# Pooling an image for attention: the second column addition moves from VectorE into TensorE's pooling matmuls

## What is computed

```python
# q (1, 12288, 128), kv (1, 384, 32, 128), w_sr (128, 128); r = 4, C = 128
kv_pool = kv.reshape(B, H // r, r, W // r, r, C).mean(axis=(2, 4))   # mean over 4x4 pixels: 96 x 8 = 768 keys
kv_flat = kv_pool.reshape(B, -1, C) @ w_sr
k = v = kv_flat
s = scale * (q @ k.transpose(0, 2, 1))
a = softmax(s)
x = a @ v
# then, with d_ff = 2048 in both:
h = x @ moe_w_in;   y = (h * clip(h + 3, 0, 6) / 6) @ moe_w_out
h = y @ moe2_w_in;  out = where(h >= 1, h, where(h <= -1, 0, (h + 1)**2 / 4)) @ moe2_w_out
```

## Time and profile before

| what | value |
|---|---|
| runs | 1310.63, 1313.53, 1312.01 us; median 1312.01 |
| profiled execution | 1311.85 us in all, span 1310.1 us |
| instructions | 17871 |
| TensorE matmul busy | 1282.6 us, 98% of the span |
| VectorE busy | 1221.4 us, 93% |
| ScalarE busy | 1141.8 us, 87% |
| GpSimd busy | 431.0 us, 33% |
| HBM | 16.84 MB read, 6.29 MB written |

### The profile page before, as it was taken

The page is one execution under the profiler, slowest core; times in us unless marked ns, Lnnn a source line. Parts: engine busy times, 40 slices in busy tenths (PEclk is TensorE's granted clock), DMA queues, the critical chain, the costliest instruction groups (busy, mean ns, idle before and its releaser), DMA issues.

```text
span 1310.1 us, 17871 instructions
## 1 busy us (share of the span) xinstructions
PE 1282.6 (98%) x5826; PEld 1071.5 (82%) x5826; DVE 1221.4 (93%) x1168; ACT 1141.8 (87%) x1314; POOL 431.0 (33%) x201
## 2 busy tenths in 40 slices
PE   7897999999999999999999999999999999999998
PEld 6785888888888888888888888888888888888876
DVE  5797999999999999999999999999999999999898
ACT  3776989989989899899899998998989989988997
POOL 1654325135143152350441522504415225132000
PEclk9998999999999999999999999999999999999999
DMA  9111220311202202202112022021120220210000
GB/s 337 19 33 32 58 57 9 65 47 19 64 18 46 56 8 64 52 12 64 24 40 56 8 64 56 8 64 30 34 57 9 62 55 2 57 37 21 9 9 17
DMA packets 118500, 58.23 MB, mean 44 GB/s; under 512 B 103104, under 2 KB 104256, under 8 KB 118208
## 3 DMA queue, kind: packets, MB, share of 16 engines
q1 hardware_dynamic: 117408, 57.64, 19.0%
q10 hardware_dynamic: 1056, 0.13, 0.1%
HBM read 16.84 MB, written 6.29 MB: 18 GB/s over the span
## 4 chain that ended last, share of the span: by engine, by line
PE 90%; DVE 6%; ACT 1%; POOL 1%; issue 1%; SPq 1%; DMA 1%; ACTq 0%
PE ps L898 37%; PE ps L874 37%; PE ps L779 7%; PE ps L766 7%; DVE g_lo L664 2%; DVE gate L658 2%; SPq L283 1%; PE ps L811 1%; PE ps L819 1%; POOL probs L343 1%; DVE negmax L570 1%; PE ps L827 0%; DMA kv_sb<-in_kv 0%; ACT gate L474 0%; DVE gate L653 0%
## 5 line engine op out<-in xcount | busy, mean ns | idle before, releaser
L664 DVE TENSOR_TENSOR g_lo<-gate,g_hi 128x1024 fp32r<-128x1024 f32 x384 | 549.5, 1431 | 7.7 <-ACT g_hi L488 7.7
L658 DVE SCALAR_TENSOR_TENSOR gate<-gate,ps 128x1024 f32<-128x1024 f32 x384 | 463.5, 1207 | 12.5 <-ACT gate L482 10.6
L488 ACT ACTIVATE g_hi<-gate 128x1024 fp32r<-128x1024 f32 x384 | 402.7, 1049 | 1.4 <-DVE gate L658 1.2
L348 POOL TENSOR_TENSOR pt_lo<-pt,pt_hi 128x1024 fp32r<-128x1024 f32 x66 | 158.8, 2407 | 623.1 <-ACT pt_hi L430 623.1
L898 PE MATMUL ps<-g_hi,w_hi 128*128 128x512 f32 x768 | 301.4, 392 | 2.7 <-DVE g_lo L664 1.3
L898 PE MATMUL ps<-g_hi,w_lo 128*128 128x512 f32 x768 | 299.5, 390 | 0.0
L898 PE MATMUL ps<-g_lo,w_hi 128*128 128x512 f32 x768 | 299.4, 390 | 0.0
L343 POOL TENSOR_TENSOR probs<-probs,rinv 128x768 f32<-128x768 f32 x96 | 223.9, 2342 | 70.4 <-DVE rinv L579 70.4
L474 ACT ACTIVATE gate<-ps 128x1024 f32<-128x1024 f32 x192 | 196.9, 1025 | 55.2 <-PE ps L874 55.1
L472 ACT ACTIVATE gate<-ps 128x1024 f32<-128x1024 f32 x192 | 196.1, 1021 | 50.5 <-PE ps L874 49.3
L482 ACT ACTIVATE gate<-gate 128x1024 f32<-128x1024 f32 x187 | 198.6, 1062 | 5.9
(11 more groups left out here) (75 smaller groups left out, 1403.2 us busy)
## 6 DMA issues: line engine op xcount, KB each, us to landing
pt<-turned_p SPq DMA_DIRECT2D x352, 96.0 KB, 2.2
out<-out_sb SPq DMA_DIRECT2D x94, 64.0 KB, 1.8
kv_sb<-in_kv SPq DMA_DIRECT2D x11, 512.0 KB, 7.9
q_in<-in_q SPq DMA_DIRECT2D x88, 64.0 KB, 2.2
w_raw<-in_moe_w_in SPq DMA_DIRECT2D x2, 1024.0 KB, 14.3
kv_sb<-in_kv SPq DMA_DIRECT2D x2, 256.0 KB, 11.9
out_sb<-in_q SPq DMA_DIRECT2D x1, 256.0 KB, 12.4
q_in<-in_q SPq DMA_DIRECT2D x1, 256.0 KB, 11.7
```

Source lines behind the costliest of these rows:

```text
L348: nc.gpsimd.tensor_tensor(piece(pt_lo, g), piece(pt, g), piece(pt_hi, g).bitcast(F32), ALU.subtract).then_inc(pt_lo_done, 1)
L488: nc.scalar.activation(g_hi[:, n % RING, :], gate[:, n % RING, :], ACT.Copy).then_inc(g_hi_done, 1)
L658: nc.vector.scalar_tensor_tensor(out=gate[:, n % RING, :], in0=gate[:, n % RING, :], scalar=6.0 if mlp == 1 else 1.0, in1=hidden, op0=ALU. ...
L664: nc.vector.tensor_tensor(g_lo[:, n % RING, :], gate[:, n % RING, :], g_hi[:, n % RING, :].bitcast(F32), ALU.subtract).then_inc(g_lo_done, 1)
```

## The change

`col_sum` and `sum_cols` go. `pool_rows` waits for `halves_summed` instead and issues, for each group, two matmuls that read the two remaining columns straight from `kv_sb` and accumulate in one place of PSUM. `keep_warm(6)` behind the parts of the first two thirds becomes `keep_warm(2)`. `values_low(0)` moves from behind `sum_halves(7)` to behind `keys_low(0)`, ahead of `sum_halves(7)`. The semaphore `cols_used` is renamed `pooled`. `keys_low(1)` and `values_low(1)` stay behind all sums.

```diff
         with ExitStack() as first:
             kv_sb = sb("kv_sb", [P, KVROWS * KVW], F32, first)
-            col_sum = sb("col_sum", [P, KVROWS, WG, C], F32, first)
...
             for j in range(KVROWS):
                 keys = slice(j * KJ, (j + 1) * KJ)
-                act.wait_ge(cols_used, j + 1)
+                act.wait_ge(pooled, j + 1)
...
-            def sum_cols(m):
-                j, g, count = parts[m]
-                part = image(m).rearrange("p (g b c) -> p g b c", b=POOL, c=C)
-                dve.wait_ge(halves_summed, m + 1)
-                nc.vector.tensor_tensor(col_sum[:, j, g:g + count, :], part[:, :, 0], part[:, :, 1],
-                                        ALU.add).then_inc(cols_summed, 1)
-
...
             for m in range(PARTS):
                 sum_halves(m)
-                if 0 < m < PARTS - 2:
-                    sum_cols(m - 1)
                 if m == 6:
                     keys_low(0)
-                if m == 7:
                     values_low(0)
-                if m == PARTS - 3:
-                    sum_cols(m)
-            sum_cols(PARTS - 2)
-            sum_cols(PARTS - 1)
             keys_low(1)
             values_low(1)
             first_q_low(0)
...
             def pool_rows(m):
                 j, first, count = parts[m]
-                pe.wait_ge(cols_summed, m + 1)
+                pe.wait_ge(halves_summed, m + 1)
                 for g in range(first, first + count):
-                    last = nc.tensor.matmul(pooled_keys(j)[:, g * rows:(g + 1) * rows], col_sum[:, j, g, :], pool_m[:],
-                                            start=True, stop=True)
+                    for e in range(2):
+                        at = j * KVW + (g * POOL + e) * C
+                        last = nc.tensor.matmul(pooled_keys(j)[:, g * rows:(g + 1) * rows], kv_sb[:, at:at + C], pool_m[:],
+                                                start=(e == 0), stop=(e == 1))
                 if first + count == WG:
-                    last.then_inc(cols_used, 1)
+                    last.then_inc(pooled, 1)
...
             for m, (j, first, count) in enumerate(parts):
                 pool_rows(m)
-                if m == PARTS - 1:
+                if j < KVROWS - 1:
+                    keep_warm(2)
+                elif m == PARTS - 1:
                     turn_first_q(0)
-                elif j < KVROWS - 1:
-                    keep_warm(6)
```

More of the change, by code:

```diff
@@ L189, in build_program @@
         const_step, const_done = sem("const_step"), sem("const_done")
-        halves_summed, cols_summed, cols_used, pooled_copied = (
-            sem("halves_summed"), sem("cols_summed"), sem("cols_used"), sem("pooled_copied"))
+        halves_summed, pooled, pooled_copied = sem("halves_summed"), sem("pooled"), sem("pooled_copied")
         kt_done, kt_hi_done, kt_lo_done = sem("kt_done"), sem("kt_hi_done"), sem("kt_lo_done")
```

## The result

The changed kernel takes 1322.37 us (median of 4 runs, 1321.56 to 1323.68) against 1311.32 us for the kernel before (4 runs, 1310.18 to 1313.53): the ratio is 1.0083, with a 95% interval of 1.0066 to 1.0101. It is 11 us slower. The forecast was 1312.9 with 1322.0 as the upper end; the time lies inside what rival 1 gave, 1321.4 to 1323.6. The profiled execution of the changed kernel is the longest of its four (1323.68 us), so the shifts read from its trace come out slightly larger than that of the medians.

The account below looks back on a forecast made before the run. TensorE, busy 98% of the span, was taken as the bound. -1.57 + 0.07 + 0.27 + 1.71 gave +0.48 us, or +1.2 with a fixed clock rise; the middle, +0.9 on 1312.01, gave 1312.9 us, range 1310.6 to 1322.0.

Parts of the forecast that it names:

- rival 1: TensorE's clock stays low through all pooling: four transposes end 9.4 us late, 1321.4 to 1323.6 us; chance 0.42, full form 0.25.
- if the clock rises with `keys_and_values(0)` as it does now: Condition of the sum: TensorE's clock rises near the first keys and values and holds, giving +0.48 us; chance 0.48.
- the slow L766 above: First scores: up to 2.2 us more if L766's first twelve passes are slow too; left out of the range.
- A fall in the last third: Last third, 3.4 us of only 32-column passes: the clock falls back there, the same loss in another place.
- Step 1: Start of TensorE: it waits only for the first sum of halves, so starts at 5.90, 1.57 us earlier.
- Step 2: First third: 40 passes for 40 take the same 8.45 us; two transposes cover less of the keys' copy, 0.07 lost.
- Step 3: Second third: 40 passes for 40 at the fast pace; two transposes cover 0.21 of the 0.48 us copy, 0.27 lost.
- Step 4: Last third: 16 more pool passes with nothing taken away cost 1.71 us; accumulation charged zero.
- Step 5: VectorE: losing 5.2 us of additions gains nothing beyond the earlier start; the moved `values_low(0)` costs zero.
- The sum of the first five steps: Prologue total: +0.48 us, or +1.2 if the clock rises at 15.93 in any case; middle +0.9.
- Rival 2: Pooling: doubled pool passes raise the clock sooner than transposes do, gaining at best 2.8 us (1309.2); chance 0.10.
- Rival 3: Last third: a quarter of the 16 passes' 1.71 us were waits for `cols_summed`; about zero or -0.3 us, within the 0.48 case.

Follow-up runs that it names:

- before_warm2: Kernel before with two transposes in place of six behind each part of the first two thirds, nothing else: 1314.78 us, ratio 1.002.
- before_fill128: Kernel before with each part's six filling transposes replaced by three real float32 matmuls of the identity with itself, six 128-column passes: 1312.53 us, ratio 1.0003.
- before_fill32: Kernel before with each part's six filling transposes replaced by three float32 matmuls with the pooling matrix, six 32-column passes: 1320.43 us, ratio 1.007.
- after_early34_w4: Changed kernel with 34 transposes ahead of the first part and four in place of two behind each part: 1313.11 us, ratio 1.0002.
- before_dup_warm2: Kernel before, column sums kept, each pool matmul issued twice without accumulating, two transposes in place of six: 1324.63 us, ratio 1.0092.
- before_values: Kernel before with only the values' low part of the first third moved ahead of the sum of part 7: 1312.16 us, ratio 0.9999.
- before_early34: Kernel before with 34 transposes ahead of the first part: 1311.21 us, ratio 0.9992.
- after_early18: Changed kernel with 18 more transposes ahead of the first part, in TensorE's wait for the first load: 1322.44 us, ratio 1.0081.
- after_warm6: Changed kernel with six transposes in place of two behind each part of the first two thirds: 1321.88 us, ratio 1.0074, runs in two groups.

## Why the prediction was wrong

- **The step that failed** is the condition of the sum, "if the clock rises with `keys_and_values(0)` as it does now", together with the 0.52 against 0.42 that I gave it. It rested on a coincidence in the earlier trace rows: L838's first pass began at 15.71 us in TensorE's timeline and the pace changed at about 15.92, so I gave its columns part of the credit. In the changed kernel keys and values ran in full at 14.62 and at 24.77 and the clock did not rise. What the runs showed in its place: the rise hangs on the filling passes. Taking four of six away is enough to lose it (before_warm2). With as many passes in the same 2.13 us a part it comes at 18.4 us when the filling ones move 128 columns and only near 34.3 when they move 32 (before_fill128, before_fill32). In the changed kernel it comes at 39 in place of 15.9; with the clock high through the pooling, 9 of the 11 us go (after_early34_w4). L838 in the timeline of the kernel before:

```profile
15.71 0.71 PE L838 MATMUL ps<-pooled_t,w_sr_sb 128*128 128x256 f32 x2
```

- **What the trace had said against it.** "TensorE was without a gap from 7.47, yet stayed slow until 15.9, so issuing alone does not raise it" was the right reading. A change that thins out wide passes should then have been taken to keep the clock low until a run showed otherwise.
- **Rival 1** priced the result well. It put the end of the four transposes at 33.6 (34.41), with 1.8 us for keys and values (2.05), 6.5 for the last third (6.67), 0.9 for the transposes (0.91) and up to 2.2 more for the scores; 0.6 was measured there (3.01 against 2.40), and 0.7 ahead of them (34.41 to 36.97 against 24.20 to 26.09), where the last third's keys, values and keep-warm transposes ran slow; the prediction had no term for these. The total of 1321.4 to 1323.6 holds the 1322.37.
- **The range** left out the upper half of that rival ("the slow L766 above") and so missed the time by 0.4 us. A case that had 0.25 of chance in its full form should have stood in it with its own upper bound. A fall in the last third, which the prediction named as the same loss in another place, was seen as well, in after_early34_w4 at about 24.7.
- **Step 1** (earlier start) was right: 6.09 against 5.90, the first load being 0.18 later in this execution. **Step 2** held: 8.53 us from the first pass to keys, against 8.45 + 0.07, with 0.08 of waiting at 14.53.
- **Step 3** held in form: 40 passes for 40, but at 0.203. Its 0.27 us for a copy that two fast transposes do not cover could not show: at the slow pace two transposes take 0.48, as long as the copy needs. No run has two transposes a part at the high pace through this third.
- **Step 4** held: 16 more passes, no charge for accumulation. before_dup_warm2 has the same pace without it, and after_early34_w4 gives 3.49 us at the high pace for the 3.42 of the forecast.
- **Step 5** held at the low pace: from 6.09 to 39.98 the chain of the changed kernel never touches VectorE. The moved values cost nothing by themselves in before_values. Behind its last sum VectorE now waits 5.88 us for keys. With the clock up the step would not hold without limit: in before_early34 TensorE waits 1.10 us for a column sum.
- **The sum of the first five steps** (+0.48 to +1.2) was never measured by itself. The nearest is after_early34_w4 beside before_early34, 1.67 us later at the first scores with 16 added transposes among them.
- **Rival 2** fell: with twice the pool passes the rise came later, not sooner. The rule named with it, in the Trainium skill, "TensorE: Matmul & The Clock Gate", Part 4 (PE-mode transpose), is that transposes do not count as TensorE being busy in the way matmuls do. The runs do not agree with it: 18 transposes alone took the clock to 2.4 GHz in after_early18, and real matmuls of equal width did no better in before_fill128. **Rival 3** fell too. In after_early34_w4 no column sums exist, and VectorE's last sum of halves ends at 21.41, 0.2 us after the last third's 32 passes began. They take 0.109 us each, against 0.107 in the kernel before, so a quarter of that 1.71 us cannot have been waits. VectorE's timeline in after_early34_w4:

```profile
20.98 0.43 DVE L598 TENSOR_TENSOR kv_sb<-kv_sb 128x256 f32<-128x256 f32 x1 [0.29 <-DMA kv_sb<-in_kv]
```

## What to carry to other kernels

Where a stage fills TensorE with passes of few columns, read its clock from the start-to-start time of like instructions, not from busy time or from a clock column that may begin late. Before removing "useless" transposes or swapping them for narrow matmuls, count the columns that they move: in before_fill32 and before_fill128 the same number of passes in the same time left the engine at half its clock until 34.3 us or until 18.4. If a change may move such a step, the step's full price belongs in the range, however well the rest of the sum is worked out.

## What was not expected of the hardware

By its pace, the clock stayed at 1.2 GHz with TensorE back to back from 6 to 39 us in the changed kernel. It fell with the engine nearly always busy: 2.91 of 3.40 us ahead of the fall in after_early18, and in after_early34_w4 after 16.40 of 16.50 us, at the end of 32 narrow passes. And one program can spread widely: after_warm6 gives 1318 to 1319 or 1325 to 1328 us, far more than the 3.7 us over which the kernel before spreads. That this is the moment of the rise is likely, but not shown.
